# Linear attention, a token-mixing gated layer and a convolution-gated layer: keys exponentiated token-major, their product with the values in one plain fp32 matmul per column block

## What is computed

```python
q_s = softmax(q, axis=-1)              # per token and head
k_s = exp(k - max_over_tokens(k)); k_s /= (sum_over_tokens(k_s) + 1e-9)
kv  = einsum('bhsd,bhse->bhde', k_s, v); x = einsum('bhsd,bhde->bhse', q_s, kv)
# gated layer (the "mix"), x is 576 x 512
h = gelu_tanh(x @ w_in); u, v = h[..., :512], h[..., 512:]
v_n = layernorm(v) * g_ln
v_s = w_sg @ v_n + b_sg[:, None]       # mixes the 576 tokens
x = x + (u * v_s) @ w_out
# last layer
h = relu(x @ w_in2); c = conv3_over_tokens(h, conv_w)
out = (h * sigmoid(c)) @ w_out2
```

## Time and profile before

| | us |
|---|---|
| three runs | 1015.23, 1016.77, 1013.86 (median 1015.23) |
| span of the profiled execution | 1014.0 |
| PE busy | 972.6 (96%) |
| DVE, ACT, POOL busy | 665.1, 408.9, 358.6 |
| one loop body of phase one (m = 1 to 6) | 68.65 |
| phase two, from its second group of matmuls at 624.0 to the end of the last one | 386.7 |

### The profile page before, as it was taken

How to read it: one execution, slowest core, us unless ns; L and a number is a source line. 1 busy time by engine, 2 the same in 40 slices (tenths; PEclk the granted TensorE clock), 3 DMA queues, 4 the chain that set the end, 5 groups by cost and what they waited for, 6 DMA issues and landing times.

```text
span 1014.0 us, 17663 instructions
## 1 busy us (share of the span) xinstructions
PE 972.6 (96%) x6816; PEld 933.1 (92%) x6816; DVE 665.1 (66%) x992; ACT 408.9 (40%) x656; POOL 358.6 (35%) x241
## 2 busy tenths in 40 slices
PE   3779999999999999999999998999999999999998
PEld 2669989999899999998999897999999999999998
DVE  8894783865856838748645678675757575757560
ACT  5454352543544434534422444343434343434331
POOL 4455264353352542634421413322222232323230
PEclk9989999999999999999999998999999999999999
DMA  7511403113104022031020241002020202020001
GB/s 252 156 53 26 157 22 122 50 31 114 57 21 137 34 83 98 26 119 57 21 82 27 89 162 47 25 20 76 12 83 13 83 12 81 12 81 12 36 19 52
DMA packets 32395, 67.40 MB, mean 66 GB/s; under 512 B 2912, under 2 KB 2912, under 8 KB 32352
## 3 DMA queue, kind: packets, MB, share of 16 engines
q1 hardware_dynamic: 27744, 57.37, 17.2%
q10 hardware_dynamic: 4608, 9.44, 2.4%
HBM read 46.87 MB, written 18.87 MB: 65 GB/s over the span
## 4 chain that ended last, share of the span: by engine, by line
PE 80%; DVE 14%; issue 3%; ACT 2%; DMA 1%; POOL 0%; DVEq 0%; SPq 0%; ACTq 0%
PE psum L383 64%; PE psum L375 8%; DVE plain_arena L1101 3%; PE psum L505 2%; DVE plain_arena L1076 2%; PE psum L431 2%; PE psum L400 2%; PE psum L412 1%; DVE plain_arena L1005 1%; DVE split_arena L1035 1%; PE psum L433 1%; ACT plain_arena L737 1%; DMA plain_arena<-in_q 1%; DVE plain_arena L1028 1%; DVE plain_arena L994 1%
## 5 line engine op out<-in xcount | busy, mean ns | idle before, releaser
L383 PE MATMUL psum<-split_arena 128*128 128x288 f32 x5568 | 764.0, 298 | 9.9 <-DVE split_arena L1139 5.2
L383 PEld LDWEIGHTS psum<-split_arena 128*128 128x128 f32 x5568 | 750.4, 190 | 16.8 <-issue 7.4
L1438 POOL TENSOR_TENSOR plain_arena<-plain_arena 128x576 f32<-128x576 f32 x64 | 107.3, 1677 | 295.3 <-ACT plain_arena L913 295.3
L375 PE MATMUL psum<-split_arena 128*128 128x512 f32 x480 | 117.4, 397 | 0.1
L1281 DVE TENSOR_SCALAR plain_arena<-plain_arena 128x576 f32<-128x576 f32 x64 | 39.9, 623 | 114.1 <-ACT plain_arena L907 114.1
L375 PEld LDWEIGHTS psum<-split_arena 128*128 128x128 f32 x480 | 89.7, 191 | 17.8 <-DVE split_arena L1062 0.4
L1286 DVE SCALAR_TENSOR_TENSOR plain_arena<-plain_arena 128x576 f32<-128x576 f32 x64 | 96.9, 1514 | 2.3
L907 ACT ACTIVATE plain_arena<-psum 128x576 f32<-128x576 f32 x64 | 41.5, 650 | 93.2 <-PE psum L383 58.7
L1349 POOL TENSOR_TENSOR split_arena<-plain_arena,split_arena 128x512 fp32r<-128x512 f32 (+1 forms) x40 | 51.4, 1286 | 75.8 <-ACT split_arena L687 75.8
L1337 POOL TENSOR_TENSOR plain_arena<-plain_arena 128x1024 f32<-128x1024 f32 (+1 forms) x24 | 39.0, 1636 | 98.6 <-DVE plain_arena L994 98.6
L1121 DVE TENSOR_TENSOR split_arena<-plain_arena,split_arena 128x576 fp32r<-128x576 f32 x32 | 24.3, 759 | 68.6 <-ACT split_arena L759 68.4
(11 more groups left out here) (71 smaller groups left out, 959.3 us busy)
## 6 DMA issues: line engine op xcount, KB each, us to landing
x_dram<-plain_arena ACTq DMA_DIRECT2D x32, 288.0 KB, 2.1
plain_arena<-x_dram SPq DMA_DIRECT2D x8, 1152.0 KB, 5.6
outT<-plain_arena SPq DMA_DIRECT2D x32, 288.0 KB, 2.1
plain_arena<-in_v SPq DMA_DIRECT2D x32, 256.0 KB, 4.2
plain_arena<-in_kT SPq DMA_DIRECT2D x7, 1152.0 KB, 8.4
plain_arena<-in_q SPq DMA_DIRECT2D x7, 1024.0 KB, 5.6
plain_arena<-in_w_in SPq DMA_DIRECT2D x8, 512.0 KB, 4.9
plain_arena<-in_w_out SPq DMA_DIRECT2D x6, 512.0 KB, 4.5
```

The source lines that it names most:

```text
L375: mm = e.matmul(out, stat[s], mov[m], start=first and n == 0, stop=last and n == 2, skip_group_check=True)
L383: mm = e.matmul(out[:, h, 0:NH], stat[s], mov[m][:, h * NH:(h + 1) * NH], start=first and n == 0, stop=last and n == 2, skip_group_check=True)
L1438: e.tensor_tensor(gt[:, f % 2, :], gt[:, f % 2, :], hp[:, f % 2, 1:T + 1], ALU.mult).then_inc(hg_full, 1)
```

## The change

- Keys now come token-major (`k`), are made exp(k - max) in place by POOL (`sub_k`, with `kmax_all`, the negated maxima on every partition) and ACT (`exp_k`), and are neither transposed nor split nor normalised. The transposed keys (`kT`) are still loaded for `max_k`; the 512 maxima go through DRAM to all partitions (`spread_kmax`: 2 KB out, 256 KB in). For batch 0 PE transposes the raw keys and spreads the maxima itself.
- `kv_piece` is one plain fp32 matmul of 130 columns per column block: 128 values and two columns of ones, which give the sum of each key column. DVE divides by it afterwards (`finish_kv`).
- The tail's v part holds hi rows and lo rows of x side by side as one stationary operand (`x_tail`), so it takes 8 matmuls where there were 12, all of them now behind the other v parts; ACT and DVE fill `x_tail`, and `copy_tail` (ACT) and `sum_tail` (DVE) add the two halves of the result before `gelu_v(m, 2)`.
- The tail step of `sg_unit` uses all 128 rows in its four matmuls.
- All hardware loops are written out.

```diff
+            def load_k(b):
+                e.wait_ge(kv_step, b * NJ)
+                e.dma_start(kn[:, 0:NJ - 1, :], k[b, 0:TF, :].rearrange("(j p) c -> p j c", p=P)).then_inc(k_in, 16)
+                e.dma_start(kn[0:TAIL, NJ - 1, :], k[b, TF:T, :]).then_inc(k_in, 16)
+            def load_kT(b):
+                if not (isinstance(b, int) and b == 1):
+                    e.wait_ge(k_neg, negs(b - 1))
+                e.dma_start(k_view, kT[b].rearrange("(p a) s -> p a s", a=DT)).then_inc(kT_in, 16)
...
+            def spread_kmax(b):
+                e.wait_ge(k_neg, negs(b))
+                e.dma_start(kmax_dram[b].rearrange("(p a) -> p a", a=DT), kmax).then_inc(kmax_out, 16)
+                e.wait_ge(kmax_out, 16 * b)
+                e.wait_ge(k_sub, NU * b)
+                e.dma_start(kmax_all, kmax_dram[b].partition_broadcast(P)).then_inc(kmax_in, 16)
...
+            def turn_raw_k(u):
...
+                for d in range(DT):
+                    for j in UNITS[u]:
+                        out = psum[:, 2 * d + j // (NJ - 1), (j % (NJ - 1)) * P:(j % (NJ - 1) + 1) * P]
+                        mm = e.transpose(out, kn[:, j, d * P:(d + 1) * P], ident)
+                    if u == NU - 1:
+                        mm.then_inc(k_raw_turned, 1)
...
-                _, keys, values = k_places(b, j)
-                at = VSP_ODD_AT if first(b, j) else VSP_AT
-                both = split_arena[0:rows, at:at + 2 * D].rearrange("p (h n) -> p h n", h=2)
                 for d in range(DT):
-                    cols = slice(d * P, (d + 1) * P)
-                    e.matmul(kv_sums[:, d, :, :], keys[0][0:rows, cols], both[:, :, cols],
-                             start=j == 0 and d % 2 == 0, stop=j == NJ - 1, skip_group_check=True)
-                    mm = e.matmul(kv_sums[:, d, 0, :], keys[1][0:rows, cols], values[0][0:rows, cols],
-                                  start=False, stop=j == NJ - 1, skip_group_check=True)
+                    mm = e.matmul(kv_sums[:, d // 2, d % 2, 0:VW], kn[:, j, d * P:(d + 1) * P], v_place(b, j)[:, d, :],
+                                  start=j == 0 and d % 2 == 0, stop=j == NJ - 1, skip_group_check=True)
                 mm.then_inc(kv_step, 1)
...
+                    if u == 2:
+                        if d == 0:
+                            e.wait_ge(x_tail_hi, b + 1)
+                            e.wait_ge(x_tail_lo, b + 1)
+                        for m in (0, 1):
+                            mm = e.matmul(tail_bank, x_tail[:, d, :], win[m][:, d, F:2 * F],
+                                          start=d == 0 and m == 0, stop=d == DT - 1 and m == 1,
+                                          skip_group_check=True)
+                        continue
...
-                    for rows, m in ((P, 0), (TAIL, 1)):
+                    for m in (0, 1):
                         for h in HALVES:
-                            mm = e.matmul(main_sets[f % 2][:, h, 0:NH], vn[0][0:rows, j, cols],
-                                          wsg[m][0:rows, j, h * NH:(h + 1) * NH], start=False, stop=m == 1,
+                            mm = e.matmul(main_sets[f % 2][:, h, 0:NH], vn[0][:, j, cols],
+                                          wsg[m][:, j, h * NH:(h + 1) * NH], start=False, stop=m == 1,
...
-                v_part(m, 2, [0, 1])
                 late = isinstance(m, int) and m == 0
                 if a is not None and not late:
-                    turn_k(a, 0)
                     turn_q(a, 0)
                 v_part(m, 0, [DT - 1])
                 v_part(m, 1, [DT - 1])
                 if late:
-                    turn_k(a, 0)
                     turn_q(a, 0)
-                v_part(m, 2, [DT - 2, DT - 1])
+                v_part(m, 2, list(range(DT)))
...
+            def exp_k(b, u):
+                t, n, rows = UNITS[u][0], len(UNITS[u]), rows_of(u)
+                e.wait_ge(k_sub, b * NU + u + 1)
+                e.activation(kn[0:rows, t:t + n, :], kn[0:rows, t:t + n, :], ACT.Exp).then_inc(k_exp, 1)
...
+            def copy_tail(b):
+                e.wait_ge(v_done, b * NU + NU)
+                e.activation(vg[0:TAIL, NJ - 1, :], tail_bank[TAIL:P, :], ACT.Identity).then_inc(v_tail_lo, 1)
...
+                hi_x_tail(m)
                 if start:
                     exp_k(a, 0)
-                    exp_k(a, 1)
-                    split_v(a, 0)
                     hi_late(W_SG, w_sg_raw, w_sg_hi[1], 1)
                     exp_q(a, 1)
                 if a is not None:
                     exp_q(a, 2)
+                    exp_k(a, 1)
+                    exp_k(a, 2)
                 if start:
                     hi_late(W_OUT, w_out_raw, w_out_hi, 1)
-                elif a is not None:
-                    split_v(a, 0)
                 gelu_v(m, 0)
                 gelu_v(m, 1)
+                copy_tail(m)
                 tile(0)
                 gelu_v(m, 2)
                 hi_vn(m, 0)
...
+            def finish_kv(b):
                 e.wait_ge(kv_step, (b + 1) * NJ)
+                sums = ksum.rearrange("p (a b) -> p a b", a=2).unsqueeze(3)
+                e.tensor_scalar(sums, kv_sums[:, :, :, P:P + 1], EPS_SOFTMAX, None, ALU.add).then_inc(k_chain, 1)
+                e.wait_ge(k_chain, 2 * b + 1)
+                e.reciprocal(krec, ksum).then_inc(k_chain, 1)
+                e.wait_ge(k_chain, 2 * b + 2)
+                if not (isinstance(b, int) and b == 0):
+                    e.wait_ge(kv_lo, 2 * b)
                 for h in HALVES:
                     at = slice(h * HD, (h + 1) * HD)
+                    scale = krec[at, :].rearrange("p (a b) -> p a b", a=2).unsqueeze(3).to_broadcast([HD, 2, 2, HD])
+                    e.tensor_tensor(kvn[at, :, :].rearrange("p (a b) n -> p a b n", a=2), kv_sums[at, :, :, at], scale,
+                                    ALU.mult).then_inc(kv_norm, 1)
             def lo_kv(b):
                 for h in HALVES:
...
+            def lo_x_tail(b):
...
+                e.tensor_copy(x_tail[:, :, TAIL:P], xT[1][:, :, TF:T]).then_inc(x_tail_lo, 1)
...
+            def sum_tail(b):
+                e.wait_ge(v_tail_lo, b + 1)
+                place = vg[0:TAIL, NJ - 1, :]
+                e.tensor_tensor(place, tail_bank[0:TAIL, :], place, ALU.add).then_inc(v_tail_sum, 1)
...
                 lo_x(m, DT - 2)
-                if start:
-                    max_k(a, 0)
-                    max_k(a, 1)
-                elif a is not None:
-                    norm_k(a)
+                if a is not None and not start:
                     sum_q(a, 0)
                 lo_x(m, DT - 1)
+                lo_x_tail(m)
                 if start:
                     max_q(a, 1)
                     max_q(a, 2)
                     sum_q(a, 0)
-                    norm_k(a)
-                if start:
                     lo_w_sg(1)
                 if a is not None:
                     sum_q(a, 1)
                     sum_q(a, 2)
                 moments(m, 0)
                 tile(0)
+                sum_tail(m)
                 moments(m, 1)
...
+            def sub_k(b, u):
+                t, n, rows = UNITS[u][0], len(UNITS[u]), rows_of(u)
+                e.wait_ge(kmax_in, 16 * b)
+                e.wait_ge(k_in, 32 * b)
+                e.tensor_tensor(kn[0:rows, t:t + n, :], kn[0:rows, t:t + n, :],
+                                kmax_all[0:rows, :].unsqueeze(1).to_broadcast([rows, n, D]), ALU.add).then_inc(k_sub, 1)
...
                     scale_q(a, 0)
-                    lo_v(a, 0)
+                    sub_k(a, 1)
                     scale_q(a, 1)
                     scale_q(a, 2)
+                    sub_k(a, 2)
                     if start:
                         lo_w_out(1)
                 inverse_deviation(m, 0)
                 inverse_deviation(m, 1)
                 lo_vn(m, 0)
                 inverse_deviation(m, 2)
-                if a is not None:
-                    lo_v(a, 1)
                 lo_vn(m, 1)
                 lo_vn(m, 2)
-                if a is not None:
-                    lo_v(a, 2)
                 for f in range(FT):
-                    if f < 2 and a is not None:
-                        lo_v(a, 3 + f)
...
-                    for u in range(NU):
-                        sub_q(n, u)
+                    sub_q(n, 0)
+                    sub_k(n, 0)
+                    sub_q(n, 1)
+                    sub_q(n, 2)
```

More of the change, by code:

```diff
@@ L360, in step @@
                 store_y(b)
-            with e.Fori(0, B - 2) as i:
+            for i in range(0, B - 2):
                 step(i)
@@ L606, in _ @@
             body(0, 1)
-            with e.Fori(1, B - 1) as i:
+            for i in range(1, B - 1):
                 body(i, i + 1)
@@ L654, in _ @@
             step(1, 1)
-            with e.Fori(1, B // 2 - 1) as k:
+            for k in range(1, B // 2 - 1):
                 step(2 * k, 0)
@@ L895, in _ @@
             body(0, 1, 2)
-            with e.Fori(1, B - 2) as i:
```

(1 more changed line is left out.)

436 lines of the change are left out of this document (197 added, 239 removed).

## The result

The changed kernel takes 1030.38 us (median of 4 runs, 1029.29 to 1031.45) against 1016.0 before on the same chip; the ratio is 1.0147, 95% interval [1.0132, 1.0162]. It is slower by 14.4 us. The forecast was 1017 in a range of 990 to 1037; the profiled execution moved by +14.6 (span 1028.6 against 1014.0), the sum had said +1.6.

What follows compares the result with a forecast made beforehand. It took PE, busy 96%, as the bound: +7.2 us for bodies 1 to 6, -1.6 for body 7 and -4.0 at the start, +1.6 on profiled 1014.0; median 1.2 above the span gives 1017, own range 1009 to 1025, overall 990 to 1037.

Steps and rivals of the forecast that it cites:

- rival (2): A plain fp32 product costs 0.36 us, 0.12 more than the pair; 140 add 17 us: 1034. Chance 0.17.
- PE's savings: Middle body: key transposes 1.9 us, v tail 0.9, token-mix tail 1.1, wait for a key split 0.46; together 4.4.
- fp32 product: Key-value product: one plain fp32 matmul takes 0.24 us, as the pair before, so no change from 4.8 us a body.
- Pause ahead of `u_unit(m, 0)`: PE waits 3.7 us a body for the first gelu, queued on ACT behind key exponentials that wait for POOL.
- rival (1): DVE's copy of `x_tail` is shut out by POOL, delaying `sum_q(a, 1)` 1.4 us: +8.4 over six bodies, 1025. Chance 0.15.
- Clock: After the pause in each body PE's clock mostly drops to 1.2 GHz, losing 2.0 us; bounds 0 and 3.
- the 0.9 us of the third gelu: Ahead of `kv_piece(a, 0)`: PE would wait 0.9 us for the third gelu, hidden while the clock is low.
- Rest of the body: Behind `u_unit(m, 0)`, 4.2 us late, savings of 3.0 follow; net +1.2 us a body, +7.2 for bodies 1 to 6.
- Body 7: Without attention it saves 2.0 us and loses perhaps 0.4 to the later third gelu: -1.6.
- Start: First x product some 6 us sooner, 2 kept through body 0, plus 2 of PE's savings: -4, between -8 and +1.
- Loops: Writing the hardware loops out changes nothing, since the branch cost PE nothing before: 0 us.
- Rival (3): POOL and DVE pass without loss, 2.8 us pause, and the clock stays up: -0.5 a body, 1003. Chance 0.15.

Runs made afterwards that it cites:

- k_early: Changed kernel with POOL's key additions and ACT's exponentials for units 1 and 2 issued at the end of the body before: 996.95 us.
- exp_late: Changed kernel with only ACT's order altered, the two key exponentials behind the v part's third gelu: 1004.52 us.
- no_x_tail: Changed kernel with the v part's 64-row tail computed as before, twelve matmuls and no copies: 1011.47 us.
- filler: Changed kernel with 23 unread 512-column matmuls put ahead of `u_unit(m, 0)`: 1025.97 us.
- k_early2: `k_early` with ACT's two moved exponentials right behind the first x product's split and the queries' maximum behind two residual additions: 1029.67 us.
- k_early2_start: `k_early2` with body 0's additions and exponentials for keys of units 1 and 2 moved behind layer-norm splits and last gelu: 1025.0 us.
- before_unrolled: Kernel before with its hardware loops written out and nothing else: 1013.40 us, ratio 0.9991.

## Why the prediction was right or wrong, point by point

The range held the time and slower had the largest chance, 0.41, but the forecast itself, 1009 to 1025 around 1017, was no change that can be measured; the sum was 13 us too small. That the range held 1030 is in part luck: above 1025 it was drawn for the dear product of rival (2), which did not happen. By its own steps:

- **PE's savings**, 4.4 us a body forecast. Right, a little small. Busy time fell by 2.62 in the after trace, although the slow clock put 2.04 on it: 4.66, and 0.47 of wait; together 5.1. A kv tile's four matmuls take 0.90 us where the pairs took 0.95, which is 0.25 of the 0.7; the rest is not placed. The token mix is shown by two experiments.
- **fp32 product**, 0.24 forecast, 0.22 measured. Right; rival (2), 0.36, is out.
- **Pause ahead of `u_unit(m, 0)`**, 3.7 us forecast, 5.52 measured. The mechanism was right link by link (`k_early` and `exp_late` take it away); the term was mis-sized. Of the 1.8 us, 1.4 is rival (1), which I had given 0.15 because before a small `tensor_scalar` had once passed unhindered; `no_x_tail` gives it as 1.44. POOL's `sub_k` is 0.49 longer on 128 rows and 0.2 on 64, and I had priced it by `sub_q`. The second operand of `sub_q` repeats one value over a head, that of `sub_k` is a full row; that this is the reason was not tested. PE itself came about 0.3 later than counted, which takes as much off the pause. This term makes 11 of the 13 us over six bodies. It was the step to bound upwards: I had written that POOL has no slack, and that 0.3 us of shift decides.
- **Clock**, 2.0 forecast, 2.04 measured, on all six bodies. Right, as is the 0.9 us of the third gelu under it (`filler`: 0.86).
- **Rest of the body.** The wait of 0.46 for the residual addition ahead of the x products was not foreseen, 2.8 us in all. It is gone in `k_early2`, where the queries' maximum stands behind these additions. The maxima and the loads of the keys are hidden, as said.
- **Body 7**, -1.6 forecast, -0.8 measured; its wait for `gelu_u` rose to 1.73 us.
- **Start**, -4 forecast, -2.0 measured, inside its bounds. The first x product came 6.65 us sooner, as forecast, and body 0 gave it back in the same queue; `k_early2_start` regains 4.7 of it.
- **Loops**, 0 forecast; confirmed within `before_unrolled`'s interval, -4 to +2 us.
- **Rival (3)**, the clock stays up, did not happen at 5.52 us, but did in four of six bodies at 3.18: with my pause of 3.7 the clock's 2.0 us would not have been certain either.

## What to carry to other kernels

An instruction that is moved into an in-order queue brings along what it waits for: list what is queued behind it, and give the chain that releases it an upper bound with every lock-out between DVE and POOL counted. If the moved step's inputs are ready long before, issue it where its engines stand idle (here the 8.8 us of POOL at a body's end), and check the order of the queue again after every such move. Work taken from the busiest engine is worth nothing in front of a wait, and can, by the copies that it needs, lengthen the wait.
